# Attention and two MLPs: the second half of the first batch moves from VectorE's band sums to TensorE, 96 tokens at a time

## What is computed

```python
# attention, per batch and head: two parts are added
q_d, k_d, v_d = means of 4 neighbouring tokens of q, k, v       # 144 pooled tokens
out_up    = repeat(softmax(q_d @ k_d.T / 8) @ v_d, 4)           # every pooled output for 4 tokens
mask      = abs(i - j) < 4                                      # a band of 7 keys per query
out_local = softmax(where(mask, q @ k.T / 8, -1e9)) @ v
x = (out_up + out_local) as [2304 tokens, 512]
# MLP 1, d_ff 2048
g = relu(x @ w_in) ** 2 ;  x = g @ w_out
# MLP 2, d_ff 768
h = max(relu(x @ w1), x @ w2, x @ w3) ;  out = h @ w_out2
```

## Time and profile before

| | |
|---|---|
| median of 3 runs | 847.05 us (846.48 to 855.23) |
| the profiled execution: its time, its span | 846.34 us, 844.6 us |
| TensorE busy | 809.7 us, 96% of the span |
| VectorE, ScalarE, GpSimd busy | 57%, 39%, 28% |
| granted TensorE clock, mean | 0.988 |
| opening, chunk 0, chunk 1 | 35.1, 79.2, 74.3 us |
| chunks 2 to 6 | 56.5, 66.3, 58.7, 64.4, 51.8 us |
| chunk 7 up to its last ReLU, then the second MLP | 46.2, 312.1 us |

### The profile page before, as it was taken

One profiled execution on the slowest core, in us unless ns is written; L12 is line 12 of the kernel. 1 busy time (PEld: TensorE's weight loads), 2 busy tenths in 40 slices (PEclk: granted clock), 3 DMA queues, 4 the chain that ended last, 5 costly groups with the idle time before them and its releaser, 6 DMA issues.

```text
span 844.6 us, 13557 instructions
## 1 busy us (share of the span) xinstructions
PE 809.7 (96%) x5568; PEld 775.4 (92%) x5568; DVE 484.9 (57%) x547; ACT 329.3 (39%) x883; POOL 237.7 (28%) x200
## 2 busy tenths in 40 slices
PE   8979879989999999999999999999999999999996
PEld 7869878989999989989999999999999999999996
DVE  5879997979978999778980028521212212122212
ACT  4656465454665455644545344211212112121111
POOL 5688941234412365213454222100000000000000
PEclk9999989999999999999999999999999999999999
DMA  8992240021410044101000045310111102010001
GB/s 176 295 273 51 55 109 15 11 64 36 122 50 8 15 93 122 30 1 41 3 30 1 1 152 165 91 63 1 38 37 32 44 1 76 1 38 1 18 21 37
DMA packets 52422, 51.01 MB, mean 60 GB/s; under 512 B 22136, under 2 KB 43912, under 8 KB 51592
## 3 DMA queue, kind: packets, MB, share of 16 engines
q1 hardware_dynamic: 49788, 49.41, 21.8%
q10 hardware_dynamic: 2572, 0.73, 0.4%
HBM read 38.63 MB, written 10.62 MB: 58 GB/s over the span
## 4 chain that ended last, share of the span: by engine, by line
PE 73%; DVE 17%; POOL 4%; ACT 2%; issue 1%; DMA 1%; SPq 1%; ACTq 0%
PE PS L628 23%; PE PS L630 22%; PE PS L629 22%; DVE tmp L1169 3%; DVE sc L1178 3%; DVE tmp L1219 2%; DVE qk L1231 2%; PE PS L653 2%; PE PS L669 2%; PE PS L821 1%; ACT x L991 1%; DVE WO L1318 1%; DMA v_tok<-v 1%; POOL G L1603 1%; PE PS L660 1%
## 5 line engine op out<-in xcount | busy, mean ns | idle before, releaser
L628 PE MATMUL PS<-XS,WI 128*128 128x288 f32 (+1 forms) x768 | 244.9, 319 | 3.7 <-POOL WI L1583 2.4
L629 PE MATMUL PS<-XS,WI 128*128 128x288 f32 (+1 forms) x768 | 239.4, 312 | 0.0
L630 PE MATMUL PS<-XS,WI 128*128 128x288 f32 (+1 forms) x768 | 239.4, 312 | 0.0
L1603 POOL TENSOR_TENSOR G<-g,G 128x288 fp32r<-128x288 f32 x128 | 148.6, 1163 | 248.5 <-ACT G L1004 248.1
L628 PE MATMUL PS<-G,WO 128*128 128x288 f32 x512 | 158.4, 309 | 6.8 <-DVE WO L1318 4.4
L628 PEld LDWEIGHTS PS<-XS,WI 128*128 128x128 f32 x768 | 145.4, 189 | 9.0 <-issue 3.1
L629 PE MATMUL PS<-G,WO 128*128 128x288 f32 x512 | 152.2, 297 | 0.0
L630 PE MATMUL PS<-G,WO 128*128 128x288 f32 x512 | 152.0, 297 | 0.0
L629 PEld LDWEIGHTS PS<-XS,WI 128*128 128x128 f32 x768 | 146.1, 190 | 1.3
L630 PEld LDWEIGHTS PS<-XS,WI 128*128 128x128 f32 x768 | 145.8, 190 | 0.0
L1501 DVE TENSOR_TENSOR t<-PS,t 128x384 f32<-128x384 f32 x36 | 20.1, 557 | 156.3 <-PE PS L630 156.3
(11 more groups left out here) (158 smaller groups left out, 1155.4 us busy)
## 6 DMA issues: line engine op xcount, KB each, us to landing
x_scratch<-x2s SPq DMA_DIRECT2D x8, 576.0 KB, 3.5
XR<-x_scratch SPq DMA_DIRECT2D x6, 768.0 KB, 4.7
qk<-q SPq DMA_DIRECT2D x7, 576.0 KB, 6.7
out<-osb SPq DMA_DIRECT2D x14, 256.0 KB
qk<-k SPq DMA_DIRECT2D x3, 1152.0 KB, 9.5
vb<-v SPq DMA_DIRECT2D x3, 1152.0 KB, 7.8
WIr<-moe_w SPq DMA_DIRECT2D x12, 256.0 KB, 3.3
WIr<-moe_w_in SPq DMA_DIRECT2D x4, 512.0 KB, 6.4
```

The costliest lines, as they stand in the source:

```text
L628: mm(dst, wt(HI), xt_(HI), start=first, stop=False)
L629: mm(dst, wt(HI), xt_(LO), start=False, stop=False)
L630: return mm(dst, wt(LO), xt_(HI), start=False, stop=last)
L1603: Q.tensor_tensor(G[:, s % NGR, LO], g32[:, s % 2], G[:, s % NGR, HI].bitcast(f32), ALU.subtract).then_inc(g_ready, 1)
```

## The change

The second 288 tokens of batch 0 take the way of the first, during the steps of chunk 0. All of it uses the two PSUM banks that the steps leave free (banks 0 and 1 of the attention's list). New tasks of batch 0 are "qF" and "kF" (transposes of q and k), "S" 3 to 5 (scores of 96 queries), "P" 3 to 5 (turned probabilities), "ps", "pt", "po" 2 and 3 (pooled scores, turned, outputs) and "out" 3 to 5. VectorE's band, the heads, "qP", the trip through DRAM and the x tasks of batch 0 go. The pooled outputs are copied by a DMA into 24 further rows of v (rows 104 to 127 of `v_blk2`), and the turned probabilities have a spreading pattern in those rows, so one matmul gives both parts. Places, exps and the weight tiles of VectorE are set anew, and so is the order of loads: the band's loads of q, k and v for batch 0 go, loads of v in blocks of 104 rows come, and q and k of batch 1 are loaded earlier.

```diff
-    QK_AT = {1: (1, 1, 3), 2: (2, 13, 1), 3: (4, 10, 2)}
-    HEADS_AT = {0: (0, 2, 2), 1: (1, 4, 0), 2: (2, 15, 3), 3: (4, 13, 1)}
+    QK_AT = {1: (1, 0, 1), 2: (2, 14, 1), 3: (4, 9, 1)}
+    HEADS_AT = {1: (1, 3, 0), 2: (3, 0, 1), 3: (4, 13, 0)}
...
+    SECOND_AT = [((0, 0, 0), ("qF", 0)), ((0, 0, 0), ("qF", 1)), ((0, 0, 2), ("qF", 2)), ((0, 0, 3), ("qF", 3)),
...
-    EXP_AT = {(0, 6): 1, (2, 0): 3, (3, 12): 5, (5, 10): 7}
+    EXP_AT = {(1, 1): 2, (2, 1): 3, (2, 15): 4, (3, 13): 5, (4, 11): 6, (5, 11): 7}
...
-    W_DVE = [9, 11, 13, 15, 17, 19, 21, 23]
+    W_DVE = [1, 3, 5, 9, 13, 17]
...
+            def second_features(which, c):
+                task = (("qF", "kF")[which], c)
+                ps = bank(task)
+                pe.wait_ge(second_loaded[which], 16 * POOL)
+                for t in range(POOL):
+                    last = nc.tensor.transpose(ps[:, UNITS * t:UNITS * (t + 1)], two_heads(second_half(which), c, t), ident[:UNITS, :UNITS])
+                full(last, task)
...
+            def block_out(i):
+                ps = bank(("out", i))
+                if i == BL:
+                    pe.wait_ge(v_blk2_loaded, 16 * BL)
+                    pe.wait_ge(od_second_loaded, 16 * BL)
+                for e in range(2):
+                    read(pe, 0, ("P", i, e))
+                for c in range(KC):
+                    for e in range(2):
+                        last = mm(ps[64 * e:64 * e + 64, QR * c:QR * (c + 1)], v_blk2[:, i % BL, 2 * c + e], probsT(i, e, c),
+                                  start=c == 0, stop=c == KC - 1)
+                full(last, ("out", i))
...
+            Q.memset(spread_behind, 1.0).then_inc(behind_made, 1)
+            pool.wait_ge(behind_made, 1)
+            Q.affine_select(out=spread_behind, in_=spread_behind, compare_op=ALU.is_ge, fill=0.0, base=POOL * (KR - 96),
+                            pattern=[[0, 2 * KC], [0, BL], [1, QR]], channel_multiplier=-POOL).then_inc(behind_made, 1)
...
             for b in range(1, NB):
                 lo, hi = FIRST[b], LAST[b]
-                dve.wait_ge(q_loaded[0], 16 * b)
-                dve.wait_ge(k_loaded, 48 * (b + 1))
-                seg = score_steps(lo, two)
-                run(seg, 4)
+                if b > 1:
+                    dve.wait_ge(q_loaded[0], 16 * b)
+                    dve.wait_ge(k_loaded, 48 * b)
+                    seg = score_steps(lo, two)
+                    run(seg, 4)
                 pool_k(b)
```

More of the change, by code:

```diff
@@ L664, in attend @@
                     read(pe, b, ("t", h))
-                    if h == 0 and b:
+                    if h == 0:
                         pe.wait_ge(vd_loaded, 32 * b)
-                    for n in halves(b):
+                    for n in range(2):
                         for kn in range(2):
@@ L729, in block_scores @@
-                if i == 0:
+                    mm(view(ps[e][:QR, :KC * KR], "p (c k) -> p c k", c=KC), ones_r,
+                       mask_r[:, which].unsqueeze(1).broadcast_to([QR, KC, KR]), start=True, stop=False)
+                if i % BL == 0:
                     for c in range(KC):
-                        read(pe, 0, ("qT", c))
-                        read(pe, 0, ("kT", c))
-                    read(pe, 0, ("kE",))
+                        for kind in (("qT", "kT"), ("qF", "kF"))[half]:
+                            read(pe, 0, (kind, c))
+                    if half:
+                        pe.wait_ge(k_edges_made, 2)
+                    else:
+                        read(pe, 0, ("kE",))
@@ L734, in block_scores @@
                 for c in range(KC):
[L735 to L736 removed]
+                    last = [mm(ps[e][:QR, KR * c:KR * (c + 1)], all_qT[half][64 * e:64 * e + 64, c, at:at + QR],
+                               all_kT[half][64 * e:64 * e + 64, c, at:at + KR], start=False, stop=c == KC - 1) for e in range(2)]
@@ L1408, in _ @@
             block_turned(2, 1)
+            second_k_edges()
             for c in range(KC):
                 first_lo_part(c)
[L1412 to L1423 removed]
@@ new lines, in next_w @@
+            def next_w():
+                split_w(next(w_tiles))
+            next_w()
+            for c in range(KC):
+                k_features("kF", c)
+            sum_q(1)
+            next_w()
+            block_lows(3)
+            next_w()
+            pooled_lows(2)
+            block_normed(3)
+            for e in range(2):
+                block_turned(3, e)
+            for e in range(2):
+                pooled_turned(2, e)
+            next_w()
+            block_lows(4)
+            dve.wait_ge(q_loaded[0], 16)
@@ new lines, in _ @@
+            dve.wait_ge(k_loaded, 48)
+            seg = score_steps(FIRST[1], two)
+            run(seg, 2)
+            pooled_lows(3)
+            block_normed(4)
+            for e in range(2):
+                block_turned(4, e)
+            next_w()
+            for e in range(2):
+                pooled_turned(3, e)
+            block_lows(5)
+            run(seg, 3)
+            for a in (2, 3):
+                second_pooled_normed(a)
+            V.memset(vb[:, 0:HALO, :], 0.0)
+            V.memset(vb[:, HALO + GL:, :], 0.0).then_inc(v_zeroed, 1)
```

523 lines of the change are left out of this document (291 added, 232 removed), and 7 rows, old and new, of tables (SECOND_AT, X_AT).

## The result

| | before | changed |
|---|---|---|
| median of 16 runs each, side by side | 847.35 us (843.56 to 856.25) | 855.83 us (854.85 to 859.24) |
| ratio, 95% interval | | 1.0083 [1.0055, 1.0111] |
| span of the profiled execution | 844.6 us | 854.9 us |
| opening | 35.1 | 36.2 |
| chunks 0 and 1 | 79.2, 74.3 | 74.1, 74.5 |

What follows compares the result with a forecast made beforehand. TensorE was taken to set the end. Chunk 0 -5.0, chunk 1 +0.1, opening +0.3 and chunks 2 to 7 -0.5 sum to -5.1 us, from the median of 847.05 to 841.9 us; 8 in 10 range 832 to 852.

Steps and rivals of the forecast that it cites:

- Chunk 0: Chunk 0 takes 51 + 17.6 added work and slow steps less removed 10.1 hidden in the old time, 5.6 waits: 74.2 us, -5.0.
- my first sign: Chunk 0's border stretch at 74 us, with no wait behind VectorE after step 12, would show the forecast right.
- my second rival: GpSimd becomes the bound of steps 9 to 15 in chunk 0: +8.7 and a clock dip of 1.7, 852.3 us; 12%.
- my term: In chunk 0, TensorE waits 1.0 us for GpSimd, which has both weight tiles of each step from step 9 on.
- line 1716 ending waits of TensorE in steps 12 to 15: Sign in chunk 0 that would show the forecast wrong; no size given.
- the rule named with the term: A VectorE instruction with two SBUF inputs holds GpSimd's port for its whole length, a reduction never; alone it makes the term about 0.
- Chunk 1: Chunk 1 changes by +0.1 us: TensorE idles 3.7 at its start plus slow clock, 7.9 us of waits against 7.8 before.
- The opening: GpSimd's three pattern instructions, 1.9 us each ahead of its sums, cost +0.3 us; bounds 0 and +3.
- Chunks 2 to 7: Batch 1's second x tasks +1.0, batch 2's qk tasks -1.5, rest 0: sum -0.5 us, bounds -6 and +6.
- Rest 0: Everything in chunks 2 to 7 besides batch 1's second x tasks and batch 2's qk tasks changes by 0.
- the lead is given back: Fixed exp places make ScalarE and TensorE wait at (2,15), (3,13), (4,11), (5,11): four times 1.5 us, 847.9 us; 14%.
- my last sign: Chunks 3 and 5 more than 3 us off would show the forecast wrong.

Runs made afterwards that it cites:

- experiment 3: The changed kernel with the exp of batch 1's second half moved from step (2,1) to (1,15): 852.78 us, 1.0039 of the kernel before.
- experiment 4: The kernel before with only the second halves' x tasks of batches 2 and 3 at the change's earlier places: 853.33 us, 1.0042 of the kernel before.
- 5: The changed kernel with batches 2 and 3 (places, exps, VectorE's order) as in the kernel before: 843.36 us, 0.9941 of the kernel before.
- 6: The changed kernel with VectorE's head maxima untied from the weighted sums, two steps behind each head: 857.33 us, 1.0113 of the kernel before.
- 9: The changed kernel with only the second exps of batches 2 and 3 two steps earlier, (3,11) and (5,9): 854.94 us, 1.0098 of the kernel before.
- 10: The changed kernel with VectorE's heads untied and the second exps of batches 2 and 3 two steps earlier: 847.29 us, 1.0002 of the kernel before.
- the last version: Changed kernel with accumulators emptied first, heads untied, second exps of batches 1 to 3 earlier, masks behind sums, batch 2's qk turn earlier: 837.23 us, 0.9893 of before.

## Why the prediction was wrong, point by point

- **Chunk 0** was right in its sum: 74.1 against 74.2. Its waits were 6.4 us where I laid out 5.6, and that they come so near is in part luck: the ones that I had listed came to 4.6, and the longest, 1.78 us at 108.13 for VectorE's pooled sums of batch 1, was not on the list and is a wait behind VectorE after step 12, which my first sign excluded. The waits for VectorE's weight tiles and for x tasks are gone. TensorE is busy for 67.7 us at full clock; before it was 65.8 with some 4.8 us of slow clock in the stretch, so some 7 us of work were added on balance, where I had 17.6 - 10.1 = 7.5.
- **GpSimd in steps 9 to 15**, my second rival, came near, and it held TensorE a little. Its 12 tiles, from 76.92 on, took 1.75 us each and the 7 squares 0.99, 27.9 us in all against my 27.1 and the rival's 35.8. From 90.91 to 107.36 GpSimd had no gap, and its tiles ended waits of 0.30 and 1.27 us, of which my term was 1.0; by my own list ("line 1716 ending waits of TensorE in steps 12 to 15") that was a sign of being wrong. The average hides two kinds of tile:

```profile
88.39 1.28 POOL L1716 TENSOR_TENSOR WO<-WOr,WO 128x512 fp32r<-128x512 f32 x1
...
98.86 2.39 POOL L1716 TENSOR_TENSOR WO<-WOr,WO 128x512 fp32r<-128x512 f32 x1
```

The first ran beside one of VectorE's sums of the band (88.95 to 90.30), the second beside a product with two inputs (98.28 to 100.11); the tiles at 95.72 and 101.98 also ran beside products and took 2.41 and 2.37. This is of the kind that the rule named with the term states. The rival's own arithmetic was off: 12 tiles and 7 squares fill 28.8 us once a tile and 7/12 of a square cost 2.4 us, not 2.1, and 35.8 is 7.0 more than 28.8, not 8.7.
- **Chunk 1** was right in sum (+0.2 against +0.1) and in its main part: a wait of 3.16 us for the emptying at 120.39 where I had 3.7, and slow clock for 6.8 us (119.2 to 126.0, the first 1.2 still in the wait), so about 2.8 lost where I had 1.7. The 3.7 was itself a slip: 10.2 to 10.5 less 6.9 is 3.3 to 3.6.
- **The opening** was +1.1 where I had +0.3, inside its bounds. The patterns cost 2.01, 2.29 and 2.29 us, near the 1.9 taken, but GpSimd's sum of k, which started at 11.38 before, started at 13.37. I had reckoned with the slack ahead of v's sum in the earlier trace rows only, and had not looked up the one ahead of k's.
- **Chunks 2 to 7**, the step that failed: sum -0.5 with bounds of 6 either way, measured +13.3 for chunks 2 to 6. I wrote "Rest 0" of the x tasks and exps of batches 2 and 3, without a reason. They had been moved 1.75 and 1 steps towards VectorE's work (from (4,5,3) to (4,4,0) and from (6,3,0) to (6,2,0)), and the exps that VectorE starts from one step away from it ((3,12) to (3,13), (5,10) to (5,11)). In the kernel before VectorE ended 3.1 us ahead of TensorE (324.12 and 327.26). What stands in place of the 0 is two waits of 3.55 and 4.65 us with their slow clock, 12.8 us in chunks 4 and 6. The gap is made between exp and x task, 25.1 us on VectorE against 21.7 on TensorE (experiment 3). Moving the x tasks alone makes such waits in the kernel before (experiment 4), setting batches 2 and 3 back removes them (5), and of the two holds on VectorE's start, the heads and the exp's place, both must go for the waits to go (6, 9 and 10). Of the rest, +2.0 and +1.4 in chunks 2 and 3 and -2.8 in chunk 5, experiment 3 moved only the wait at 240.29.
- My sentence that VectorE "has its lead only up to the exp of (2,1)" was borne out: VectorE stands 8.28 us there. I drew from it that nothing changes behind, where it said the opposite: with no lead left, every place behind it counts by itself, and places had been changed.
- **Rival "the lead is given back"** was right in naming the exps' fixed places and wrong in how they act. ScalarE stands in front of its squares at (2,15), by 1.60 us, as the rival had it. At (3,13) it hardly waits and VectorE hardly either (0.38 us), at (5,11) VectorE waits 3.57; both times the start is late for the x tasks, which the rival did not see. Priced at 6 us it would have had to be 13. Nor did my last sign, chunks 3 and 5 more than 3 us off, catch it: they were off by 1.4 and 2.8, and the loss was in 4 and 6.

The numbers: with the failed term at +13.3, and the opening at +1.1 and the second MLP at +0.8, the sum of the working gives 846.3 - 5.1 + 0.2 + 1.1 + 13.3 + 0.8 = 856.6. All five are measured stretches, so that this is the profiled execution's time shows only that nothing is left out. What makes the second MLP 0.8 us longer no run shows.

## What to carry to other kernels

Where the order of work is written out as places, read each pair of places between which one engine works alone, from where it is released to where its result is fetched, and hold its length on both engines against each other: such a pair costs its difference however much lead the engine had before, as long as the place, and not the engine itself, sets the start. An engine that waits anywhere has no lead to spend, so work taken off it ahead of that point gains nothing behind it. When a wait goes and the time doesn't, look for the next handover of the same pair of engines, and for edits that only pay together.

## What the runs showed that I had not expected

The clock's answer to a short wait differs from one kernel to the next. Early in chunk 5 TensorE waits 1.55 us for ScalarE in the changed kernel and in ten of the others, always for the same copy. In the changed kernel and six others the clock stayed at its upper level; in four it fell to 1.2 GHz for 3.4 us, in the last version from 370.1 to 373.5. The rows of the two kernels' chunk 5, of the changed kernel first:

```profile
376.10:437.60 61.50, 59.95 (x482) 58.86 (x481) 47.75 (x46) 29.23 (x86) 25.91 (x19) 1.00 0.05 16
```

```profile
362.79:425.68 62.89, 61.34 (x483) 60.25 (x482) 50.71 (x48) 29.28 (x86) 27.21 (x19) 0.97 0.05 15
```

So chunk 5 is 61.5 to 61.6 us or 62.9 to 63.0 in these eleven kernels and nothing between. The Trainium skill ("TensorE: Matmul & The Clock Gate", section "Part 1: The HAM clock gate", under "What's actually happening") says that the gate's observation runs free of the kernel; the rows agree, in that the same wait at another time has another result. Of the 35 waits of 2.38 us and more in the traces, 34 had half clock with them, for 3.4 us or for 6.8; the one without is the 2.43 us at 300.60 in the fifth experiment. Two waits of 1.26 us had it as well, beginning 1.9 us behind them. A difference of 1.4 us between two of these kernels can be this alone.
